# Loads of a kernel's head split over two DMA queues: every second piece of q and k issued by ScalarE

## The reference

```python
def _attn_ref(q, k, v, tau) -> np.ndarray:      # q, k, v: (2, 6016, 256)
    qn = q / (np.linalg.norm(q, axis=1, keepdims=True) + 1e-06)
    kn = k / (np.linalg.norm(k, axis=1, keepdims=True) + 1e-06)
    s = kn.transpose(0, 2, 1) @ qn / tau
    s = s - s.max(-1, keepdims=True)
    a = np.exp(s)
    a /= a.sum(-1, keepdims=True) + 1e-09
    return (v @ a).astype(np.float32)

def _moe_ref(x, w_in, w_out, alpha) -> np.ndarray:   # w_in (256, 2048), w_out (2048, 256)
    h = x @ w_in
    g = np.maximum(h, 0.0) + alpha * np.minimum(h, 0.0)
    return (g @ w_out).astype(np.float32)
```

## Time and profile before

| | us |
|---|---|
| median of 3 runs (lowest, highest) | 1109.07 (1108.78, 1109.29) |
| the profiled execution's own time | 1105.99 |
| its span, first to last instruction | 1104.2 |
| TensorE busy | 1088.7 (99%) |
| VectorE busy | 863.7 (78%) |
| ScalarE busy | 629.9 (57%) |

### The profile page before, as it was taken

The page is one execution under the profiler, slowest core; times in us unless marked ns, Lnnn a source line. Parts: engine busy times, 40 slices in busy tenths (PEclk is TensorE's granted clock), DMA queues, the critical chain, the costliest instruction groups (busy, mean ns, idle before and its releaser), DMA issues.

```text
span 1104.2 us, 13485 instructions
## 1 busy us (share of the span) xinstructions
PE 1088.7 (99%) x4876; PEld 911.1 (83%) x4876; DVE 863.7 (78%) x1365; ACT 629.9 (57%) x1034; POOL 3.1 (0%) x10
## 2 busy tenths in 40 slices
PE   8989999999999999999999999999999999999998
PEld 7867878888888888888899888888888888888897
DVE  5878997777877777787787977877877877787675
ACT  5665666555555655665666655655655555655544
POOL 1000000000000000000000000000000000000000
PEclk9999999999999999999999999999999999999999
DMA  9720012122113101102101001101101001100100
GB/s 369 298 95 5 27 65 77 39 77 93 42 39 96 39 1 34 39 1 77 49 29 39 34 1 39 39 1 39 39 1 39 38 1 34 39 1 1 39 1 34
DMA packets 19860, 56.45 MB, mean 51 GB/s; under 512 B 1873, under 2 KB 6993, under 8 KB 18129
## 3 DMA queue, kind: packets, MB, share of 16 engines
q1 hardware_dynamic: 19792, 55.59, 14.1%
HBM read 43.26 MB, written 12.32 MB: 50 GB/s over the span
## 4 chain that ended last, share of the span: by engine, by line
PE 90%; DVE 5%; DMA 2%; ACT 1%; issue 1%; SPq 0%; ACTq 0%; DVEq 0%
PE y_ps L422 45%; PE x_ps L398 22%; PE z_ps L398 11%; PE p_ps L398 6%; PE s_ps L348 3%; PE p_ps L390 2%; DVE acc L847 2%; DMA v_stage<-v_t 2%; DVE h L818 1%; DVE h L826 1%; ACT h L602 1%; DVE g_lo L833 1%; PE p_ps L370 0%; DVE acc L759 0%; PE y_ps L390 0%
## 5 line engine op out<-in xcount | busy, mean ns | idle before, releaser
L602 ACT ACTIVATE h<-x_ps,sigma 128x512 f32<-128x512 f32 (+1 forms) x384 | 261.3, 681 | 316.4 <-PE x_ps L398 302.0
L422 PE MATMUL y_ps<-g_hi,w_hi 128*128 128x512 f32 (+1 forms) x768 | 297.3, 387 | 0.0
L422 PE MATMUL y_ps<-g_hi,w_lo 128*128 128x512 f32 (+1 forms) x768 | 296.5, 386 | 0.0
L422 PE MATMUL y_ps<-g_lo,w_hi 128*128 128x512 f32 (+1 forms) x768 | 296.4, 386 | 0.0
L612 ACT CAST g_hi<-h 128x512 fp32r<-128x512 f32 (+1 forms) x384 | 234.1, 610 | 80.6 <-DVE h L826 72.0
L826 DVE SCALAR_TENSOR_TENSOR h<-h,alpha_sb 128x512 f32<-128x512 f32 (+1 forms) x384 | 273.7, 734 | 0.0
L818 DVE SCALAR_TENSOR_TENSOR h<-z_ps,sigma,h 128x512 f32<-128x512 f32 (+1 forms) x192 | 141.8, 739 | 166.7 <-ACT h L602 166.6
L833 DVE TENSOR_TENSOR g_lo<-h,g_hi 128x512 fp32r<-128x512 f32 (+1 forms) x384 | 250.0, 672 | 6.4 <-ACT g_hi L612 6.4
L422 PEld LDWEIGHTS y_ps<-g_hi,w_hi 128*128 128x128 f32 x768 | 144.4, 188 | 29.2 <-DVE g_lo L833 1.1
L422 PEld LDWEIGHTS y_ps<-g_hi,w_lo 128*128 128x128 f32 x768 | 144.4, 188 | 27.4
L422 PEld LDWEIGHTS y_ps<-g_lo,w_hi 128*128 128x128 f32 x768 | 144.5, 188 | 26.9
(11 more groups left out here) (91 smaller groups left out, 822.5 us busy)
## 6 DMA issues: line engine op xcount, KB each, us to landing
stage<-qk SPq DMA_DIRECT2D x11, 1024.0 KB, 14.2
v_stage<-v_t SPq DMA_DIRECT2D x20, 512.0 KB, 4.5
y_t<-y_stage SPq DMA_DIRECT2D x20, 512.0 KB, 2.8
pair<-qk SPq DMA_DIRECT2D x18, 512.0 KB, 3.6
pair<-w_in SPq DMA_DIRECT2D x12, 256.0 KB, 4.8
late<-qk SPq DMA_DIRECT2D x2, 1024.0 KB, 14.3
y_stage<-w_out SPq DMA_DIRECT2D x4, 512.0 KB, 4.8
v_stage<-v_t SPq DMA_DIRECT2D x4, 448.0 KB, 4.0
```

The costliest lines, as they stand in the source:

```text
L422: product = nc.tensor.matmul(y_ps[t][oc][:, 0:H], w_part[:, j, ws], g_part[:, k, 0:H], start=jp == 0 and k < 2 and w_part is w_hi and g_pa ...
L602: nc.scalar.mul(h[:, k, 0:H], X[:, 0:H], sigma[:, j:j + 1]).then_inc(x_copied, 1)
```

## The change

The first seven loads are shared between two queues. SyncE issues p0, p2, the two small loads, p4, p6, the tile of v, and then everything as before. ScalarE issues p1, p3 and p5 as its first instructions, ahead of its wait for the constants. No wait, buffer or piece size changes, and no arithmetic.

```diff
@@ in the block of SyncE
-            for i in range(RING):
+            for i in range(0, RING, 2):
                 load_piece(i)
-                if i == 1:
+                if i == 2:
                     sp.dma_start(tau_sb[:, :], tau[:, :]).then_inc(small_loaded, 16)
                     sp.dma_start(alpha_sb[:, :], alpha[:, :]).then_inc(small_loaded, 16)
             load_v(0)
@@ in the block of ScalarE
+            for i in range(1, RING, 2):
+                n0, n1 = START[i], START[i] + PIECES[i]
+                act.dma_start(stage[:, i, 0:PIECES[i], :].rearrange("p n c -> p (n c)"),
+                              qk[0, :, n0 * ROW:n1 * ROW]).then_inc(stage_loaded[i], 16)
             act.wait_ge(const_ready, 5)
             nc.scalar.activation(warm[:, :], ones[:, 0:1], ACT.Sqrt)
```

## The result

| | us |
|---|---|
| after, median of 7 runs (lowest, highest) | 1112.95 (1110.54, 1113.98) |
| before, median of 7 runs beside them | 1108.78 (1106.35, 1109.29) |
| ratio after to before, 95% interval | 1.0039 (1.0026 to 1.0053) |
| the profiled execution's own time, and its span | 1112.41, 1110.6 |

The change costs 0.39%, about 4.3 us. In the new file VectorE's and ScalarE's lines stand four lower from the insertion on (L847 is L851), TensorE's and SyncE's as before.

The account below looks back on a forecast made before the run. The prediction took TensorE, busy 99% of the span, as the bound, with loads mattering only in the head, where VectorE's and TensorE's chains end together. VectorE +3.2 and clock +1.3 gave +4.5: 1109.07 to 1113.6 us, range 1108.0 to 1115.5.

Parts of the forecast that it names:

- Small loads, the deciding step: Head: VectorE adds nothing before alpha lands; bounded by two sharing rules, alpha was put at 15.7 us instead of 8.47.
- Turns by rows: Two loading queues alternate row by row, so tiny rows give way to 8 KB rows; alpha lands at 15.3 to 16.0.
- the dip: Loads fall to 135 GB/s from 6.0 to 7.2 us: the small rows last 1.2 us, each costing a slot.
- one load's share per packet: Alternative grain of the queues' turns: order p0, p1, p2, p3, tau, p5, alpha, giving the same 15 to 16 us.
- VectorE's sum: Head: first addition at 16.2, VectorE's end at 51.3 against 48.08, +3.2 us at TensorE's channel sums.
- v's stall: VectorE's 4.28 us of idling until v landed at 23.46; claimed to go wholly, as v is there before ScalarE asks.
- Hidden parts: Head: ScalarE's three issues, about 1.3 us, lie in its idle time, and the big pieces arrive in time; cost 0.
- TensorE's clock: Behind an idle time of 4.1 us before the channel sums, TensorE's clock falls; +1.3 us, bounds 0 and 1.7.
- the stretch at 85: Before's slow TensorE stretch behind 2.24 us of idling: 1.2 GHz level for about 3.4 us, some 1.5 us lost.
- shared by bytes or in one order: Rival: alpha lands at 10 to 12.2, v decides as before; 1108.2 to 1109.3 us; chance 0.38.
- the one with a late ScalarE queue: Rival: table load first, p1 lands at 9.7, TensorE's run ends 0.9 later; up to 1115.5 us; chance 0.02.
- the faster one: Rival: head gains 0.87 us and the slow stretch at 85.68 goes, 1.5; -2.4 in all, 1106.7 us; chance 0.05.

Follow-up runs that it names:

- e2: Against after, the two small loads stand behind p0, one load earlier in SyncE's queue; 1111.01 us, ratio to before 1.0039.
- e3: Against e2, ScalarE's three pieces go as six loads with rows of 4 KB instead of 8 KB; 1106.85 us, ratio to before 1.0002.
- e1: Against before, all loads stay in SyncE's one queue and only the small loads move behind the third piece; 1106.21 us, ratio 1.0002.
- e4: Against after, VectorE's wait for the small loads, with sigma and tau_inv, stands behind its thirteenth addition; 1105.88 us, ratio to before 0.9998.
- e6: Against after, the two small loads stand first of all in SyncE's queue, ahead of p0; 1111.37 us, ratio to before 1.0034.
- e5: Against after, 17 matmuls of zeros fill TensorE's idle time ahead of the channel sums; 1108.98 us, ratio to before 1.0018.
- e7: Against before, one queue, with the tile of v issued behind the fifth piece instead of the seventh; 1106.92 us, ratio 0.9991.
- e8: Against e7, two warming matmuls instead of six, and ten zero matmuls in group 1's idle time; 1104.85 us, ratio to before 0.9976.

## Why the prediction was right

By its own steps, against the trace of after:

- **Small loads, the deciding step.** Turns by rows were taken, alpha at 15.7: measured 15.46. The rule itself was an assumption of the prediction, since no row of before showed two loading queues: the dip that it was chosen by says what a small row costs within one queue, not how two queues share. So the choice was in part luck. e2 and e3 show the rule (12.70 and 8.73, both in the interval computed beforehand, and 155 packets against 156), and e1 shows that one place further back in one queue does not do it.
- **The Trainium skill's page "DMA: Bandwidth & Descriptors".** In the Trainium skill, section "Queues, rings and completion order" of this page has an engine go round the queues packet by packet. Read as one load's share per packet it fitted after as well; e2 refutes that reading (10.3 against 12.70 measured), and the grain here is the row. Section "Issuing engines are not separate DMA queues" of the same page of the Trainium skill says that a second issuing engine saves only issue time. The bandwidth agrees (418 GB/s around 10 us in after, 419 in the earlier trace rows), and e4 agrees in time (0.9998); as a forecast of no change it was wrong, because it speaks of the sum of the bytes and not of who in a queue waits for whom.
- **VectorE's sum.** First addition 16.2, measured 15.94; last 51.3, measured 50.89; v's stall gone wholly. +3.2 us predicted at the channel sums, +2.81 measured.
- **Hidden parts.** ScalarE's issues took 1.38 us and ended ahead of the table load (1.3 predicted). p0 to p12 were in time in after. What the prediction missed, though it did not bear on after: a row behind the small loads in the same queue is as late as they are. In after that is p4, wanted at 19.3; in e2 it was p2, and in e6 p0.
- **TensorE's clock, the mis-sized term.** +1.3 was taken within 0 and 1.7; the trace shows 3.34 us, twice the upper bound. The place and the sign were right, and e5 shows that the idle time is its cause. The size was read from the stretch at 85, where TensorE went on with full matmuls and the low level lasted some 3.4 us. At 51 it lasted to 58.3: 3 us of one-column matmuls came first, and after them the engine did another four at half speed. Whether the one-column matmuls made it last longer was not tested. The upper bound should have been the whole work up to the next known full-speed row.
- **Total.** 4.5 us predicted, 6.15 in the two traces at L398, 4.3 by the ratio of the runs. The difference between the last two lies in before: its profiled execution (1105.99) was under all of its seven timed ones. The profiles of the kernels differ in whether the clock falls behind the idle times of 2.07 and 2.24 us, and the mean granted clocks of the runs go with the times of before in the later batches: about 1104.7 us at 0.999, 1107.1 to 1108.0 at 0.997 and 1110.0 at 0.995 (averages of each batch). At the same mean clock after, measured in a batch of its own, is 2.5 to 2.7 us longer (1110.9 at 0.996, 1112.7 at 0.995), which is about the 2.81 us of the head. By the medians, then, the clock adds only some 1.5 us to it, because before often has its own slow stretches. That +4.5 missed the 4.3 by only 0.2 us is therefore in part luck: the two traces differ by 6.15 us, and the median of before lay above its trace.
- **Small slips.** The two small loads are 8.5 KB, not 8.6. The range of the forecast itself, 1111.6 to 1115.5, is wider than its terms, which give some 2.8 to 5.2 us (alpha at 15.3 to 16.0, clock 0 to 1.7), 1111.9 to 1114.3. The end of TensorE's run was put at 47.26, the modelled end of its last matmul; the next one can start 0.2 us earlier (47.05 in e7).

The rival "shared by bytes or in one order" fell with alpha at 15.46, the one with a late ScalarE queue with the issues at 0.73, and the faster one because the head's end moved back and the slow stretch behind 91.83 stayed.

## What to carry to other kernels

Before loads are spread over two queues, follow the small ones: each short row gives way to a long row of the other queue, and so does all that stands behind it in its own. In one saturated queue the same small loads cost about 1.2 us of the stream. A wait for a small operand belongs in front of its first reader, not in front of the loop. Where two chains end together, shortening one gains no more than its lead over the other (3 us gave 1.08 in e7). And an idle time of TensorE is to be priced with the slow stretch that may follow it: here 3.97 us cost another 3.3, and even 2.07 us was followed by one in some executions.

## What the runs showed of the hardware

- Two hardware queues of one core took turns row by row while both had work: between 9 and 12 us of e2 the trace has 156 packets of one and 155 of the other, and sums with one row of 8 KB or 4 KB for each small row give alpha's time within 0.5 us in after, e2 and e3. In e6, where the small rows were the first of all, they would give 8.5 and 7.27 was measured.
- In the profiled executions, an idle time of 2.07 us on TensorE left the clock full in before, after, e1 and e7 and brought a stretch at the 1.2 GHz level in e2 to e6 and e8; one of 2.21 to 2.24 us did so in before, after, e1, e2, e4 and e5 and not in e3, e6 and e7. What decides between them is open. One of 3.97 us cost 3.3 us in after, and behind one of 3.79 us ahead of p0 TensorE's run began with some 4 us at half rate in e6. In e2 the clock stayed full behind the stop of 2.62 us at 12.9, with records of 0.218 us from 15.53 on.
- The time of an execution goes with its mean granted clock: before went from 1104.7 us at a mean granted clock of 0.999 to 1110.0 at 0.995.
